# Decay attention, top-1 experts and a tanh MLP in one launch: a gathered tile turned in halves, more dummy products, the last two units mixed by token tile

## The reference

```
attention   q, k, v: 2 x 8 heads x 768 x 64; blocks of 64 positions, per head a decay lam
            out = (q k^T * lam^(i-j), lower triangle) v  +  (q * lam^(i+1)) state
            state = lam^64 * state + (k * lam^(63-i))^T v
x           1536 tokens x 512
experts     logits = x @ w_gate (8 experts); e = argmax; gate = softmax(logits)[e]
            y = gate * (relu(x @ w1[e]) @ w2[e])        w1: 512 x 1024, w2: 1024 x 512
last layer  h = y @ w_in (512 x 2048); g = h - tanh(h); result = g @ w_out (2048 x 512)
```

## Time and profile before

| | us |
|---|---|
| three runs without a profile | 541.13, 540.94, 538.23 (median 540.94) |
| the profiled execution | 545.5, its span 543.7 |
| PE busy in the span | 516.3 (95%) |
| DVE, POOL, ACT busy | 366.3, 317.3, 262.3 |
| longest chain, share of PE | 87% |
| granted TensorE clock, mean | 0.986 |

### The profile page before, as it was taken

How to read it: one execution, slowest core, us unless ns; L and a number is a source line. 1 busy time by engine, 2 the same in 40 slices (tenths; PEclk the granted TensorE clock), 3 DMA queues, 4 the chain that set the end, 5 groups by cost and what they waited for, 6 DMA issues and landing times.

```text
span 543.7 us, 10934 instructions
## 1 busy us (share of the span) xinstructions
PE 516.3 (95%) x3974; PEld 458.5 (84%) x3975; DVE 366.3 (67%) x539; ACT 262.3 (48%) x484; POOL 317.3 (58%) x263
## 2 busy tenths in 40 slices
PE   5999959999899999999999999999999999999994
PEld 4999849999899999999878888888888888888883
DVE  7455444564436555365379999989997775997771
ACT  1244515655557666565455455545534444443431
POOL 4866056644344444454379898976855553875553
PEclk9999988999899999999999999999999999999998
DMA  8788636567576767766270000000100000100001
GB/s 321 249 287 287 202 115 186 205 196 204 181 222 203 230 184 224 243 184 214 89 276 1 1 1 1 1 1 25 54 1 1 0 1 1 59 20 2 0 1 77
DMA packets 32410, 64.56 MB, mean 119 GB/s; under 512 B 3696, under 2 KB 7792, under 8 KB 32368
## 3 DMA queue, kind: packets, MB, share of 16 engines
q1 hardware_dynamic: 30448, 57.71, 32.4%
q0 software_dynamic: 1920, 6.29, 3.5%
HBM read 57.69 MB, written 6.29 MB: 118 GB/s over the span
## 4 chain that ended last, share of the span: by engine, by line
PE 87%; DMA 4%; DVE 3%; issue 2%; ACT 2%; POOL 1%; SPq 1%; ACTq 0%; DVEq 0%; POOLq 0%
PE bank L315 26%; PE bank L317 25%; PE bank L316 25%; DMA wst<-in_w_dram 3%; PE bank L1129 2%; PE bank L1104 2%; PE bank L1115 2%; PE bank L1150 1%; PE bank L1212 1%; PE bank L1141 1%; PE bank L1157 1%; POOL out_dram L644 1%; DMA x_sorted<-token_rows,tokid 1%; ACT x_h L744 1%; PE bank L1287 1%
## 5 line engine op out<-in xcount | busy, mean ns | idle before, releaser
L603 POOL TENSOR_TENSOR w_l<-wst,w_h 128x512 fp32r<-128x512 f32 x64 | 84.0, 1313 | 93.6 <-ACT w_h L723 93.5
L652 POOL TENSOR_SCALAR big<-h_sq 128x512 uint8<-128x512 f32 x48 | 79.8, 1663 | 37.4 <-ACT h_sq L797 37.1
L665 POOL TENSOR_TENSOR g_l<-g,g_h 128x512 fp32r<-128x512 f32 x48 | 63.7, 1327 | 46.0 <-ACT g_h L807 46.0
L315 PE MATMUL bank<-xs_h,w_h 128*128 (+1 forms) x256 | 72.2, 282 | 4.2 <-DVE xs_l L1012 1.4
L315 PE MATMUL bank<-wo_h,g_h 128*128 128x512 f32 x192 | 75.4, 392 | 0.0
L317 PE MATMUL bank<-wo_l,g_h 128*128 128x512 f32 x192 | 75.1, 391 | 0.0
L316 PE MATMUL bank<-wo_h,g_l 128*128 128x512 f32 x192 | 74.6, 389 | 0.0
L317 PE MATMUL bank<-x_l,win_h 128*128 128x512 f32 x188 | 74.3, 395 | 0.0
L315 PE MATMUL bank<-h_h,w_h 128*128 128x232 f32 x256 | 71.9, 281 | 2.1 <-DVE h_l L1003 1.9
L315 PE MATMUL bank<-x_h,win_h 128*128 128x512 f32 x188 | 73.9, 393 | 0.0
L316 PE MATMUL bank<-x_h,win_l 128*128 128x512 f32 x188 | 73.7, 392 | 0.0
(11 more groups left out here) (146 smaller groups left out, 1111.0 us busy)
## 6 DMA issues: line engine op xcount, KB each, us to landing
wst<-in_w_dram SPq DMA_DIRECT2D x128, 256.0 KB, 3.1
qk_in<-in_qk_t_dram SPq DMA_DIRECT2D x12, 512.0 KB, 5.4
kv_in<-in_kv_dram SPq DMA_DIRECT2D x12, 512.0 KB, 4.5
win<-in_w_in_dram SPq DMA_DIRECT2D x8, 512.0 KB, 4.5
wo<-in_w_out_dram SPq DMA_DIRECT2D x8, 512.0 KB, 7.8
token_rows<-x_sb SPq DMA_DIRECT2D x12, 256.0 KB, 4.2
x_sorted<-token_rows,tokid POOLq DMA_INDIRECT x12, 4.3
out_dram<-rows,tokid POOLq DMA_INDIRECT x12, 3.1
```

The costliest lines, as they stand in the source:

```text
L315: pe.matmul(dst, lh, rh, start=start, stop=False, skip_group_check=True)
L603: pool.tensor_tensor(w2_l[:, j % STG], wst2[:, j % STG], w2_h[:, j % 2].bitcast(F32), ALU.subtract).then_inc(w2l_ready, 1)
L652: pool.tensor_scalar(big[:, f % 2], h_sq[:, f % 2], T * T, None, ALU.is_ge).then_inc(big_ready, 1)
L665: pool.tensor_tensor(g_l[:, f % 2], g[:, f % 2], g_h[:, f % 2].bitcast(F32), ALU.subtract).then_inc(gl_ready, 1)
```

## The change

It has three parts.

1. Tile 1 is turned by its own function, `turn_in_halves`. Its transposes for features 0 to 255 go to bank 7, those for 256 to 511 to bank 5, and each pair raises a semaphore of its own. ACT and DVE take each half by an instruction of half the width, and the first `first_product` waits for the first half before its matmuls 1 to 6, and for the second half before 7 to 12. Tile 1 no longer counts in `turned`, `xsh_ready` and `xsl_ready`, so the counts of the later tiles are one lower.
2. The 13 dummy products become 20, and three more stand between the turning of tile 0 and that of tile 1.
3. The last two units (46 and 47: f = 14 and 15 of the last chunk) are no longer issued one after the other but mixed by token tile: (tile, unit) = (0,46) (1,46) (0,47) (2,46) (1,47) (3,46) (2,47) (3,47). Their low parts g_l are made by DVE instead of POOL: that of unit 46 stands in DVE's order between unit 47's last polynomial step and its `copy_predicated`, that of unit 47 after everything else of unit 47. PE waits on a new semaphore, `gl_last`, for them.

The diff, without the declarations of semaphores:

```diff
-            keep_awake(pe, 13)
+            keep_awake(pe, 20)
...
+        k_halves = [slice(0, KT // 2), slice(KT // 2, KT)]
+        tr_halves = [tr_bank(1)[:, k_halves[0]], bank[:, 5, :].rearrange("p (k t) -> p k t", k=KT)[:, k_halves[1]]]
...
+            def turn_in_halves(t):
+
+                pe.wait_ge(gathered[t], 16)
+                for k in range(KT):
+                    i = pe.transpose(tr_halves[k // (KT // 2)][:, k % (KT // 2)], x_sorted[:, t, k * P:(k + 1) * P], ident[:])
+                    if k % (KT // 2) == KT // 2 - 1:
+                        i.then_inc(half_turned, 1)
...
+                    if by_halves and k % (KT // 2) == 0:
+                        pe.wait_ge(half_low, k // (KT // 2) + 1)
...
-            turn(range(2))
-            pe.wait_ge(xsl_ready, 2)
-            first_product(0, 0, 0)
+            turn(range(1))
+            keep_awake(pe, 3)
+            turn_in_halves(1)
+            pe.wait_ge(xsl_ready, 1)
+            first_product(0, 0, 0, by_halves=True)
...
 (ACT)
-            take(range(2))
+            take(range(1))
+            for n, ks in enumerate(k_halves):
+                act.wait_ge(half_turned, n + 1)
+                act.copy(xs_h[:, ks, P:2 * P], tr_halves[n]).then_inc(half_high, 1)
...
 (DVE)
-            take(range(2))
+            take(range(1))
+            for n, ks in enumerate(k_halves):
+                dve.wait_ge(half_high, n + 1)
+                dve.tensor_tensor(xs_l[:, ks, P:2 * P], tr_halves[n], xs_h[:, ks, P:2 * P].bitcast(F32),
+                                  ALU.subtract).then_inc(half_low, 1)
...
+            def g_low(f, unit):
+
+                dve.wait_ge(gh_ready, unit + 1)
+                dve.tensor_tensor(g_l[:, f % 2], g[:, f % 2], g_h[:, f % 2].bitcast(F32),
+                                  ALU.subtract).then_inc(gl_last, 1)
...
+                if unit == LAST2 + 1:
+                    g_low(f - 1, unit - 1)
                 dve.wait_ge(big_ready, unit + 1)
...
+            g_low(FT - 1, LAST2 + 1)
             outputs(NCH - 1)
...
 (POOL)
-                    pool.wait_ge(gh_ready, unit + 1)
-                    pool.tensor_tensor(g_l[:, f % 2], ...).then_inc(gl_ready, 1)
+                    if unit < LAST2:
+                        (the same two lines)
...
 (PE)
+            def last_outputs():
+
+                pe.wait_ge(gl_last, 1)
+                for i, f in [(0, FT - 2), (1, FT - 2), (0, FT - 1), (2, FT - 2), (1, FT - 1), (3, FT - 2), (2, FT - 1),
+                             (3, FT - 1)]:
+                    if (i, f) == (0, FT - 1):
+                        pe.wait_ge(gl_last, 2)
+                    m = tile2(i, f)
+                    if f == FT - 1:
+                        m.then_inc(out_done, 1)
...
-            for unit in range(len(units)):
+            for unit in range(LAST2):
                 if unit + AHEAD < len(units):
                     hidden2(*units[unit + AHEAD])
                 output2(*units[unit])
+            last_outputs()
```

More of the change, by code:

```diff
@@ L63, in decay_attention_moe_kernel @@
     WP = F2 // E
+    LAST2 = NCH * FT - 2
     OV_KNOWN = 7
@@ L249, in decay_attention_moe_kernel @@
         xsl_ready = sem("xsl_ready")
+        half_turned = sem("half_turned")
+        half_high = sem("half_high")
+        half_low = sem("half_low")
         pad_ready = sem("pad_ready")
@@ L284, in decay_attention_moe_kernel @@
         gl_ready = sem("gl_ready")
+        gl_last = sem("gl_last")
         even_rows_out = sem("even_rows_out")
@@ L663, in _ @@
                         is_big((f + 1) % FT, unit + 1)
-                    pool.wait_ge(gh_ready, unit + 1)
-                    pool.tensor_tensor(g_l[:, f % 2], g[:, f % 2], g_h[:, f % 2].bitcast(F32),
-                                       ALU.subtract).then_inc(gl_ready, 1)
+                    if unit < LAST2:
+                        pool.wait_ge(gh_ready, unit + 1)
+                        pool.tensor_tensor(g_l[:, f % 2], g[:, f % 2], g_h[:, f % 2].bitcast(F32),
+                                           ALU.subtract).then_inc(gl_ready, 1)
                     if n and 1 <= f <= TPC:
@@ L734, in take @@
                 for t in tiles:
-                    act.wait_ge(turned, t + 1)
+                    act.wait_ge(turned, max(t, 1))
                     act.copy(xs_h[:, :, t * P:(t + 1) * P], tr_bank(t)).then_inc(xsh_ready, 1)
-            take(range(2))
+            take(range(1))
+            for n, ks in enumerate(k_halves):
+                act.wait_ge(half_turned, n + 1)
+                act.copy(xs_h[:, ks, P:2 * P], tr_halves[n]).then_inc(half_high, 1)
             def y_out(done, off, side, earlier):
@@ L1010, in take @@
                 for t in tiles:
-                    dve.wait_ge(xsh_ready, t + 1)
+                    dve.wait_ge(xsh_ready, max(t, 1))
                     dve.tensor_tensor(xs_l[:, :, t * P:(t + 1) * P], tr_bank(t),
                                       xs_h[:, :, t * P:(t + 1) * P].bitcast(F32), ALU.subtract).then_inc(xsl_ready, 1)
-            take(range(2))
+            take(range(1))
[3 more added lines that the diff above has]
+                                  ALU.subtract).then_inc(half_low, 1)
             def y_out(high, off, side):
@@ L1209, in turn @@
                     pe.wait_ge(gathered[t], 16)
-                    ge(pe, xsl_ready, t - 1)
+                    ge(pe, xsl_ready, t - 2)
                     for k in range(KT):
@@ L1213, in turn, with first_product @@
                     i.then_inc(turned, 1)
-            def first_product(off, j, unit):
+            def turn_in_halves(t):
[4 more added lines that the diff above has]
+                        i.then_inc(half_turned, 1)
+            def first_product(off, j, unit, by_halves=False):
                 pe.wait_ge(w1h_ready, unit + 1)
@@ L1243, in expert @@
                         if first:
-                            pe.wait_ge(xsl_ready, NT)
+                            pe.wait_ge(xsl_ready, NT - 1)
                             pe.wait_ge(pad_ready, 2)
@@ L1299, in hidden2, with tile2 @@
                 i.then_inc(hidden_done, 1)
+            def tile2(i, f):
+                sl = slice(i * P, (i + 1) * P)
+                return three(pe, bank[:, 4 + i, :], g_h[:, f % 2, sl], g_l[:, f % 2, sl], wo_h[:, f], wo_l[:, f],
+                             f == 0, f == FT - 1)
+            def last_outputs():
[7 more added lines that the diff above has]
+                        m.then_inc(out_done, 1)
             def output2(n, f):
@@ L1309, in output2 @@
                         pe.wait_ge((even_rows_out, odd_rows_out)[i % 2], 2 * (n - 1) + i // 2 + 1)
-                    sl = slice(i * P, (i + 1) * P)
-                    m = three(pe, bank[:, 4 + i, :], g_h[:, f % 2, sl], g_l[:, f % 2, sl], wo_h[:, f], wo_l[:, f],
-                              f == 0, f == FT - 1)
+                    m = tile2(i, f)
                     if f == FT - 1:
```

## The result

The changed kernel took 536.77 us (median of ten runs, 535.63 to 538.80); the kernel before, 541.04 us (ten runs, 538.23 to 543.88). The ratio is 0.9917, with a 95% interval of 0.9898 to 0.9937: 4.5 us, between 3.4 and 5.5. The forecast was 536.8.

A forecast was written before the change was run, and what follows sets the result against it. PE, busy 95% of the span, bounds the kernel, so only its idle or half-clock time can be won. 3.15 + 0.95 = 4.1 us off the median 540.94 gives 536.8 us, range 535.0 to 540.0.

The forecast's parts named there:

- The way in: Parts 1 and 2, up to the experts: halves and dummies together win 3.15 us.
- The first product: Start of the experts: tile 1 in halves lets PE start at 79.6 instead of 80.80, 1.2 us.
- The steps of the first products: First expert matmuls, 81.2 to 85.2 us: 19 steps at full clock instead of half win 1.95 us.
- two patterns of pauses: PE's idle times at 69.5 to 71.5 us (clock stayed) and around 140 us (clock fell), used to bound the new pattern.
- Arrival at the other end: From the first expert on: the 3.15 us carry through; tile 3's gather may cost 0 to 0.6, taken as 0.
- all which follows is driven by PE: First expert: PE's progress sets weight loads, POOL's low parts of w2 set gathers 6 to 11; six gathers are exempt.
- The end: Part 3, units 46 and 47 and the four stores: last store 0.95 us earlier, bounds 0.45 and 1.25.
- The clock falls all the same: Rival before the experts: PE starts 0.9 us earlier but at half clock, 539.5 us; chance 0.15.
- the rule on transposes: Skill page's claim that transpose-mode work does not count as busy for the clock; it would make tile turning idle time.
- the transfers take part of it back: Rival in the experts: gathers no earlier cost 0.6 us and a pause costs half clock, 538.4 us; chance 0.13.
- the end gives nothing: Rival at the last units: PE loses another 1 us, tile 0 is no earlier, 537.8 us; chance 0.07.
- The slower one: Rival before the experts: dummies run at half clock, PE starts 3.3 us later, 543.3 us; chance 0.05.

The follow-up runs named there:

- e3_dummies: The kernel before with 20 dummies and three more between tiles 0 and 1, tile 1 turned whole: 539.05 us, ratio 0.9955.
- e2_tail: The kernel before with only the mixed order of the last two units and DVE's low parts: 541.31 us, ratio 0.9987.
- e1_front: The kernel before with the halves and all dummies, its last units as before: 537.75 us, ratio 0.9929.
- e6_long: The changed kernel with 36 dummies instead of 20: 538.98 us, ratio to the kernel before 0.9957.
- e7_pool: The changed kernel with the low parts of units 46 and 47 on POOL, mixed order kept: 537.62 us, ratio to the kernel before 0.9912.
- e5_transposed: The changed kernel with its added dummy products replaced by identity transposes, two for each: 536.74 us, ratio to the kernel before 0.9896.
- f3_gate: The changed kernel with two dummy products before the attention's last gate logits: 537.29 us, ratio to the kernel before 0.9911.

## Why the prediction was right, point by point

**The way in: 3.15 forecast, 3.20 measured.** The first product: 1.2 us earlier forecast, 1.15 measured. The prediction puts this term down to the halves, and that is wrong for half of it: *e3_dummies* has 0.55 of it without them, through tile 1's transposes at full clock. By cause, the traces give 2.6 us to the dummies (and so the clock) and 0.6 to the halves. The steps of the first products: 1.95 against 2.05, the distance from the first product to tile 2 having gone from 4.81 to 2.76 us. The dummies cost nothing, with 0.66 us left where I had 0.5. The three between the tiles had nothing to spare: their records end at 77.64 and tile 1 starts at 77.66. That the clock would stay up was argued from two patterns of pauses; it is shown by *e3_dummies* against *e2_tail* (0.50 in that trace from 80 to 84 us) and by the mean clocks of the runs, though not for every run (below).

**Arrival at the other end: 0 lost forecast.** *e1_front* shows it: 3.2 us earlier made the kernel 3.8 faster (2.5 to 5.2). Tiles 2 and 3 were turned without a wait. That all which follows is driven by PE is too strong all the same: of *e6_long*'s 2.5 us later only 0.9 to 1.7 arrived in its trace, 1.4 to 2.2 by the ratios.

**The end: 0.95 forecast, 0.83 measured.** PE's wait of 0.3 us was right. Two small sizes were off. The first matmul after the wait took 0.34 us to the next instead of 0.23, and store 1 waited for DVE's copy of tile 1 and came 1.47 us behind store 0, not 1.40. `copy_predicated` took 0.73, not 1.0, which changed nothing, since ACT was held by unit 45's output as forecast (g_h starts 0.25 us behind unit 46's output, 0.26 before). What I had not said is that three quarters of this gain, 0.63 of 0.83 us, hang on DVE's shorter subtraction; *e7_pool* showed it.

**The time.** 536.8 came from subtracting 4.1 from the median of three; the median of ten is 541.04, so there was nothing to correct. That it fits to 0.1 us is luck: the interval is 2 us wide.

**The rivals.** "The clock falls all the same" is excluded for most runs, and the rule on transposes, by which it would have been the case, did not hold in *e5_transposed*; "the transfers take part of it back" by *e1_front*, whose 2.5 us at least are more than the 1.55 that this rival leaves the way in; "the end gives nothing" by the traces. The slower one, the dummies at half clock, was put at 0.05 because the clock read 1.00 from 70 to 72 us. Its mechanism exists: *f3_gate*'s trace has it for a part of the dummies. Its entry is 11.98 us, nearly the 12.40 of before. Even so that execution took 538.4 us, not 543.3, since the clock came back within the dummies. One trace of before was not evidence enough for "the clock is up here".

## What to carry to other kernels

Where PE waits for a DMA and then has dense work, look at the clock behind the wait first. Here filling the waits with dummy products up to the landing gave 2.4 us, shortening the next wait alone 0.4 (-0.7 to 1.6), and both together 3.8. Count the dummies by the landing and no further: 16 more cost 1.4 to 2.2 us. Where the end is bound by a chain of stores, finish the first tile first, put its last operand on the faster engine and use it in the last product.

## What was not expected

- **Transposes hold the clock as well as products do here.** 5.2 us of nothing else, 1.00 (*e5_transposed*).
- **The same pauses can bring the clock down or not.** 0.7, 0.34 and 0.34 us of standing between short products left it at 1.00 in all of the 13 traces but one.
- **One profiled execution can lie 4.5 us from the median.** The trace of before did, with a second stretch of half clock and longer waits for weights. Distances between two events of one trace agreed much better from kernel to kernel (the old end 8.38, 8.39, 8.37, 8.39; the entry with the whole way in 9.16 to 9.32 in seven traces, but 11.98 in *f3_gate*'s, where the clock fell, and 11.70 with the 36 dummies of *e6_long*), and settle terms that the timing of whole runs can't.
